# Chained weight loads, a scan behind the logits' transposes, and another order for the sixth unit, in a fused attention and mixture-of-experts kernel

## The chip, the core and the metric

The kernel runs on one core of one Trainium2 chip. The metric is the device time of one launch in microseconds (us), the median of several runs. The core has five engines with a queue of instructions each: PE (TensorE, matmuls), DVE (VectorE), ACT (ScalarE), POOL (GpSimd) and SP (SyncE, which here only issues DMAs). Each takes its own instructions in order and waits on semaphores for the others.

## The reference

Three stages run one after the other, all in float32:

```python
for t in range(S):                       # attention: 4 batches, 8 heads, 768 steps, head size 48
    cur = np.einsum('bhd,bhe->bhde', u[None] * kt, vt)
    y[:, :, t] = np.einsum('bhd,bhde->bhe', rt, state + cur)
    state = wt[:, :, :, None] * state + np.einsum('bhd,bhe->bhde', kt, vt)
# first MLP: 3072 tokens, 384 -> 2048 -> 384
h = x @ w_in
g = h * np.clip(h + 3.0, 0.0, 6.0) / 6.0
x = g @ w_out
# soft mixture: 8 experts with 4 slots each, 384 -> 1024 -> 384
logits = x @ phi
d = softmax(logits, over the tokens);  slot_input = d.T @ x
slot_out[e] = np.maximum(slot_input[e] @ w1[e], 0.0) @ w2[e]
out = softmax(logits, over the slots) @ slot_out
```

## The kernel before

**Units and steps.** The attention is cut into 24 units of 128 time steps of one batch: unit n is chunk n // 4 of batch n % 4. Units 0 to 3 are done ahead of the main loop. The main loop has 96 steps s. Step s does one 128-row tile of the first MLP's hidden layer for a group of four units (512 tokens): g, i = divmod(s, 16), so there are six groups of 16 tiles. Each step has nine matmuls of 512 columns on PE (`mlp`), a relu on ACT (`relu_step`), a product on DVE (`gate`) and a 32x32 block transpose of the product on DVE (`turn_gated`). Between them run four phases of one attention unit per four steps: unit 5 begins in step 1, unit 6 in step 5, and so on to unit 23.

**One unit.** DVE scans the decays from behind (`scan_suffix`) and from the front (`scan_prefix`, behind a small reciprocal, `restart_prefix`). POOL multiplies keys and receptances with them (`decay_keys`, `decay_receptance`), PE makes the scores (`score`), DVE masks them (`mask_scores`), ACT rounds them to 16 bits (`high_scores`), POOL takes the rest (`low_scores`), and PE applies them (`attend`). DVE splits the values (`low_v`) and sums the diagonal (`sum_diag`), POOL applies that (`diag_values`), DVE ends the unit (`finish_y`), and PE transposes the result for the MLP (`turn_x`). Two halves of w_in's rounding rest are made by DVE's `low_w`, the others by POOL's.

**A border.** When a group ends, its logits are folded on PE (`fold_logits`), DVE takes their maximum (`group_maximum`), ACT makes the weights, DVE transposes these (`turn_weight`) and the logits (`turn_logits`), and PE gathers the group into the slots (`gather_slots`, 64 small matmuls). DVE then adds the result up (`add_slots`), which the next group's second `score` waits for. The borders that still carry a unit are those in steps 18, 34, 50 and 66; the fifth, in step 82, carries none.

**What sets the order.** Everything is written out by hand: each engine's block has a loop over s with conditions on the phase, and an engine does its instructions in just that order. SP has one queue for all loads. Behind the last unit's rows it waits for the last `turn_x` and issues w_out and three of the second mixture's W1 tiles at once:

```python
            sp.wait_ge(x_turned, UNITS)
            sp.dma_start(att[:, 0:2 * UNIT], w_out).then_inc(w_out_in, 16)
            for e in range(2, 5):
                sp.dma_start(w1_place[e], w1[e]).then_inc(w1_in[e // 4], 16)
            sp.wait_ge(dg_ready, 16 * (C - 1))
```

w_out is read by PE behind the last group, W1 behind that. The memory that they go into is that of the attention, which is free from then on.

Of the kernel before, what the change touches and what calls it, by code (L numbers as in the profile page):

```python
# [27 lines left out]
C = S // P  # L28
# [20 lines left out]
def build_program(nc, wT, rkT, nat_in_dram, u, u_blocks, w_in, w_outT, w_out, phi, w1, w2, out):  # L49
    with ExitStack() as ctx:  # L50
# [293 lines left out]
        def is_unit(n):  # L344
            return 0 <= n < UNITS
# [10 lines left out]
        def _(sp):  # L356
# [50 lines left out]
                load_rows(n)  # L407
                load_nat(n)
            sp.wait_ge(x_turned, UNITS)
            sp.dma_start(att[:, 0:2 * UNIT], w_out).then_inc(w_out_in, 16)  # L410
            for e in range(2, 5):
                sp.dma_start(w1_place[e], w1[e]).then_inc(w1_in[e // 4], 16)
            sp.wait_ge(dg_ready, 16 * (C - 1))
            for a in range(2):
                sp.dma_start(early[a], w2[EARLY][:, a * UNIT // 2:(a + 1) * UNIT // 2]).then_inc(w2_early_in, 16)
# [42 lines left out]
        def _(pe):  # L458
# [332 lines left out]
                for a in range(4):  # L791
                    fold_earlier(a, half)
            pe.wait_ge(logits_done, C)
            pe.wait_ge(w_out_in, 16)
            for half in range(2):
                for a in range(4):
                    fold_last(a, half)
# [99 lines left out]
        def _(dve):  # L897
# [81 lines left out]
            def low_v(n):  # L979
                dve.wait_ge(v_hi_done, n - B + 1)  # L980
                nc.vector.scalar_tensor_tensor(v_lo[n % 2], nat_of(n, 2), V_SCALE, v_hi[n % 2],  # L981
                                               ALU.mult, ALU.subtract).then_inc(v_lo_done, 1)
# [10 lines left out]
            def gate(s):  # L993
                dve.wait_ge(relu_done, s + 1)
                if s >= GATED:
                    dve.wait_ge(l_ready, 4 * ((s - GATED) // 4 + 1))
                nc.vector.scalar_tensor_tensor(gated_tile(s), relu_tile(s), 6.0 * GATE, hid[s % 2][:],  # L997
                                               ALU.min, ALU.mult).then_inc(gated_done, 1)
# [135 lines left out]
            scan_suffix(B + 1)  # L1134
            restart_prefix(B + 1)
            mask_first(B)
            low_v(B)

            for s in range(END):
                n, phase = unit_of(s)  # L1140
                g, i = divmod(s, FT)
                if s <= 1:
                    gate(s)
                    turn_gated(s)
                if phase == 0:
                    if is_unit(n - 1):
                        finish_y(n - 1)
                    if n - 1 < LAST_INC:
                        add_state(n - 1)
                if phase == 1:  # L1150
                    if 1 <= g < C and i == 2:
                        group_maximum(g - 1)
                    if is_unit(n):
                        mask_scores(n)
                    if is_unit(n + 1):
                        scan_suffix(n + 1)
                        restart_prefix(n + 1)
                    if is_unit(n - 1) and n % B == 0 and n > B:
                        low_x(n - 1)
                    if 1 <= g < C and i == 2:  # L1160
                        turn_weight(g - 1)
                        turn_logits(g - 1)
                    if g == C and i == 2:
                        last_maximum()
                if phase == 2:
                    if g == C and i == 3:
                        turn_weight(C - 1)
                    if g >= 1 and i == 3:
                        sum_weight(g - 1)
                    if is_unit(n - 1) and n % B:  # L1170
                        low_x(n - 1)
                    if is_unit(n):
                        sum_diag(n)
                        low_v(n)
                if s == 0:
                    low_w(1)
                    sum_diag(B)
                if phase == 3:
                    if is_unit(n + 1):
                        scan_prefix(n + 1)  # L1180
                    if s == STEPS + 4:
                        dve.wait_ge(run_sum_done, C)
                        nc.vector.tensor_scalar(run_sum, run_sum, 1e-9, None, ALU.add).then_inc(sum_inv_step, 1)
                        dve.wait_ge(sum_inv_step, 1)
                        nc.vector.reciprocal(run_sum, run_sum).then_inc(sum_inv_step, 1)
                        dve.wait_ge(sum_inv_step, 2)
                        nc.vector.tensor_scalar(fold_inv[:], fold32, run_sum, None, ALU.mult).then_inc(fold_inv_done, 1)
                        dve.wait_ge(fold_inv_done, 1)
                        nc.vector.tensor_scalar(fold_alpha, fold_inv[:], alpha, None, ALU.mult).then_inc(fold_inv_done, 1)
                    if 1 <= g < C and i == 4:  # L1190
                        add_slots(g - 1)
                if s == 4:
                    dve.wait_ge(w_phi_ready, 4)
                    nc.vector.transpose(w_phi[:], l_ps[:]).then_inc(w_phi_done, 1)
                if s == STEPS - 12:
                    cols, tiles = c_parts[0]
                    dve.wait_ge(logits_done, C - 1)
                    nc.vector.tensor_reduce(cmax[:, tiles], by_slot(soft[:, cols]), AX_X, ALU.max).then_inc(c_max_done, 1)
                if s == STEPS - 8:
                    c_inverse(0)  # L1200
                if s == STEPS + 3:
                    copy_cT(1)
                    copy_cT(0)
                if 1 < s < STEPS - 1:
                    gate(s)
                if 1 < s < STEPS - 2:
                    turn_gated(s)
                if s == STEPS - 1:
                    last_gate(0)
                    turn_gated(STEPS - 2)  # L1210
                    last_gate(1)
                    turn_gated(STEPS - 1)
# [270 lines left out]
        def _(pool):  # L1483
# [33 lines left out]
            def low_scores(n):  # L1517
                pool.wait_ge(scores_hi_done, n - B + 1)
                nc.gpsimd.tensor_tensor(scores_lo, scores, scores_hi, ALU.subtract).then_inc(scores_lo_done, 1)  # L1519
# [56 lines left out]
            decay_keys(B + 1)  # L1576
            diag_products(B)
            low_scores(B)
            diag_values(B)

            for s in range(END):
                n, phase = unit_of(s)
                if phase == 0 and is_unit(n):
                    diag_products(n)
                if phase == 1:
                    if is_unit(n):
                        low_scores(n)
                if phase == 2:
                    if n + 1 < UNITS:
                        decay_keys(n + 1)  # L1590
                if phase == 3:
                    if n + 1 < UNITS:
                        decay_receptance(n + 1)
                    if is_unit(n) and n > B:
                        diag_values(n)
                    if n + 1 < UNITS:
                        decay_state(n + 1)
                c = split_behind(s)
                if c is not None:
                    low_w(c)  # L1600
# [73 lines left out]
```

## Time and profile before

| | us |
|---|---|
| median of 3 runs | 425.11 (424.63 to 426.47) |
| the profiled execution | 428.58 |
| its span, first to last instruction | 426.9 |
| PE busy in it | 404.4 |
| DVE busy | 338.4 |
| POOL busy | 188.1 |
| ACT busy | 162.3 |

Busy time of PE counts overlapping matmuls once, and the ends of matmuls are modelled. A profile has each instruction with its start and duration; the time in brackets behind one is what its engine idled just before it, and what is named there ended the idling. "issue" stands where the profile shows nothing that the engine waited for. The profiled execution is 3.47 us over the median of the runs without a profile.

### The profile page before, as it was taken

Reading aid. Unit: us, or ns where it says so; the run is one execution under the profiler, and the core shown is the slowest. Engines: PE = TensorE matmul, PEld = TensorE weight load, DVE = VectorE, ACT = ScalarE, POOL = GpSimd, SP = SyncE. Lnnn points to the kernel's source line nnn. Section 1 sums busy time; section 2 is a strip of 40 time slices with the busy share of each in tenths; the row PEclk is TensorE's granted clock in tenths of the full one; section 3 lists DMA queues with packets and bytes.
Section 4 is the critical chain, followed back from the end, with each engine's and each line's share of the span. In section 5 each row is a group of like instructions: output and inputs, shape, how many; then the busy total and the mean of one; then the engine's idle time right before and its main releaser. Section 6 shows DMA issues by size and latency. Waiting matters only on the chain.

```text
span 426.9 us, 9784 instructions
## 1 busy us (share of the span) xinstructions
PE 404.4 (95%) x3914; PEld 220.9 (52%) x3914; DVE 338.4 (79%) x559; ACT 162.3 (38%) x297; POOL 188.1 (44%) x178
## 2 busy tenths in 40 slices
PE   8998899999999999999999999989999699999981
PEld 4884455555555555556555555445554244543430
DVE  7897799998998989988989988898875847661242
ACT  3586256534234344234441433333333134321242
POOL 4545988874556563465555374725520012010000
PEclk9999999999999999999999999999999989999996
DMA  8999321468033313313440233121009925679929
GB/s 226 321 403 303 124 78 45 122 257 273 11 120 122 97 41 109 122 24 98 122 122 21 103 122 114 51 80 57 2 22 403 382 82 190 211 256 414 401 96 357
DMA packets 16397, 69.35 MB, mean 162 GB/s; under 512 B 2144, under 2 KB 2912, under 8 KB 14688
## 3 DMA queue, kind: packets, MB, share of 16 engines
q1 hardware_dynamic: 16352, 68.73, 46.6%
q8 instruction: 31, 0.51, 0.5%
q14 instruction: 14, 0.11, 0.1%
HBM read 64.00 MB, written 4.72 MB: 161 GB/s over the span
## 4 chain that ended last, share of the span: by engine, by line
issue 34%; PE 31%; POOL 20%; DMA 5%; DVE 5%; ACT 1%; SPq 1%; POOLq 0%; DVEq 0%
POOL att L1528 5%; PE hid L568 4%; PE hid L569 4%; PE hid L570 4%; POOL att L1492 4%; POOL att L1490 3%; DMA att<-rkT_dram 3%; POOL att L1513 3%; POOL att L1546 3%; PE hid L834 2%; PE l_ps L675 2%; POOL w_split L1504 2%; PE y_ps L534 1%; PE hid L815 1%; PE sc_ps L815 1%
## 5 line engine op out<-in xcount | busy, mean ns | idle before, releaser
L1339 ACT ACTIVATE relu<-hid,three 128x512 f32<-128x512 f32 x95 | 65.2, 686 | 142.5 <-PE hid L570 142.2
L568 PE MATMUL hid<-x_split,w_split 128*128 128x512 f16 x285 | 109.0, 382 | 3.2 <-issue 2.8
L569 PE MATMUL hid<-x_split,w_split 128*128 128x512 f16 x285 | 108.6, 381 | 0.0
L570 PE MATMUL hid<-x_split,w_split 128*128 128x512 f16 x285 | 108.5, 381 | 0.0
L997 DVE SCALAR_TENSOR_TENSOR gated<-relu,hid 128x512 f32<-128x512 f32 x95 | 64.5, 679 | 27.9 <-ACT relu L1339 27.2
L1018 DVE STREAM_TRANSPOSE ring<-gated 128x512 f32<-128x512 f32 x96 | 68.3, 711 | 3.3
L1519 POOL TENSOR_TENSOR att<-att 128x1024 f16<-128x1024 f32 x20 | 40.6, 2030 | 48.3 <-ACT att L1274 48.3
L568 PEld LDWEIGHTS hid<-x_split,w_split 128*128 128x128 f16 x285 | 27.8, 98 | 40.1 <-issue 8.5
L1537 POOL TENSOR_TENSOR att<-att 112x512 f32<-112x512 f32 x19 | 22.5, 1183 | 57.0 <-DVE att L916 57.0
L570 PEld LDWEIGHTS hid<-x_split,w_split 128*128 128x128 f16 x285 | 28.0, 98 | 34.2 <-issue 0.8
L569 PEld LDWEIGHTS hid<-x_split,w_split 128*128 128x128 f16 x285 | 28.0, 98 | 25.3 <-issue 0.9
L534 PE MATMUL y_ps<-att 112*128 112x96 f32 x160 | 33.7, 295 | 1.9 <-DVE att L981 1.4
L1528 POOL TENSOR_TENSOR att<-att 112x512 f32<-112x512 f32 x21 | 26.8, 1277 | 10.3 <-DVE att L904 10.3
L470 PEld LDWEIGHTS sc_ps<-att 48*128 48x128 f32 x384 | 23.3, 187 | 11.9 <-issue 11.8
L904 DVE TENSOR_TENSOR_SCAN att<-att 112x517 f32<-112x517 f32 x22 | 28.2, 1280 | 1.5 <-DMA att<-wT_dram 1.3
L470 PE MATMUL sc_ps<-att 48*128 48x128 f32 x384 | 27.9, 284 | 1.3 <-issue 1.3
L675 PE MATMUL l_ps<-ring,soft 32*32 32x512 f32 x192 | 25.4, 594 | 3.0 <-DVE logits L1037 2.2
L534 PEld LDWEIGHTS y_ps<-att 112*128 112x128 f32 x160 | 24.9, 189 | 6.5 <-issue 4.8
L1297 ACT ACTIVATE x_split<-y_ps 128x384 f16<-128x384 f32 x24 | 11.8, 491 | 42.1 <-PE y_ps L551 42.1
L916 DVE TENSOR_TENSOR_SCAN att<-att 112x517 f32<-112x517 f32 x22 | 26.5, 1205 | 0.0
L675 PE MATMUL sc_ps<-ring,soft 32*32 32x512 f32 x384 | 26.1, 598 | 0.0
L1274 ACT ACTIVATE att<-att 128x1024 f16<-128x1024 f32 x20 | 21.1, 1057 | 12.0 <-DVE att L936 11.0
(269 smaller groups left out, 760.2 us busy)
## 6 DMA issues: line engine op xcount, KB each, us to landing
att<-nat_dram SPq DMA_DIRECT2D x20, 576.0 KB, 4.2
att<-rkT_dram SPq DMA_DIRECT2D x22, 448.0 KB, 5.7
att<-wT_dram SPq DMA_DIRECT2D x22, 226.2 KB, 4.8
att<-w_dram SPq DMA_DIRECT2D x3, 1536.0 KB, 16.8
out_dram<-w_split SPq DMA_DIRECT2D x12, 384.0 KB, 3.9
att<-w_dram SPq DMA_DIRECT2D x5, 768.0 KB, 10.2
stage<-w_in_dram SPq DMA_DIRECT2D x2, 1536.0 KB, 15.5
ring<-w_outT_dram SPq DMA_DIRECT2D x1, 3072.0 KB, 17.1
```

What stands on the lines that cost most here:

```text
L470: last = pe.matmul(sc_bank[j][:, cols], k_dec[n % 2][rows, cols], r_dec[n % 2][rows, cols], start=True, stop=True)
L534: pe.matmul(both, r_dec[n % 2][0:PD, p * P:(p + 1) * P], state[b][0:PD, p, :], start=True, stop=False, skip_group_check=True)
L568: pe.matmul(hid[s % 2][:], high, x_high, start=(q == 0), stop=False)
L569: pe.matmul(hid[s % 2][:], high, x_low, start=False, stop=False)
L570: last = pe.matmul(hid[s % 2][:], low, x_high, start=False, stop=(q == KT - 1))
L675: ins = pe.matmul(dg_bank[a][SLOTS * c:SLOTS * (c + 1), :], weight_T[SLOTS * a:SLOTS * (a + 1), b * SLOTS:(b + 1) * SLOTS], ring_group(g, ...
L904: nc.vector.tensor_tensor_scan(suffix[0:PD, ::-1], w_rows_of(n)[0:PD, ::-1], mark[0:PD, ::-1], 1.0, ALU.mult, ALU.add).then_inc(suffix_don ...
L997: nc.vector.scalar_tensor_tensor(gated_tile(s), relu_tile(s), 6.0 * GATE, hid[s % 2][:], ALU.min, ALU.mult).then_inc(gated_done, 1)
L1018: nc.vector.transpose(ring_tile(s), gated_tile(s)).then_inc(gated_turned, 1)
L1339: nc.scalar.activation(relu_tile(s), hid[s % 2][:], ACT.Relu, bias=three[:], scale=GATE / H_SCALE)\
L1519: nc.gpsimd.tensor_tensor(scores_lo, scores, scores_hi, ALU.subtract).then_inc(scores_lo_done, 1)
L1528: nc.gpsimd.tensor_tensor(dst, keys, decay, ALU.mult).then_inc(k_dec_done, 1)
```

## The change

It has four parts.

- **Loads.** w_out is loaded in two halves, and each of the two halves and each of three W1 tiles is issued only when the one before has landed. The wait of `apply_w_out` on PE counts both halves.
- **Borders.** In steps 18, 34, 50 and 66 DVE transposes the weights and logits ahead of the next unit's `scan_suffix` and `restart_prefix`, not behind them.
- **Fifth border.** In step 82 DVE takes the group's maximum ahead of the transpose of step 81's gated tile.
- **Unit 5.** Its `scan_prefix` goes ahead of the main loop on DVE, `low_v(4)` behind the first `gate`, `sum_diag(4)` ahead of `low_w(1)`; on POOL its `decay_receptance` goes ahead of `diag_values(4)`.

```diff
             sp.wait_ge(x_turned, UNITS)
-            sp.dma_start(att[:, 0:2 * UNIT], w_out).then_inc(w_out_in, 16)
+            for half in range(2):
+                cols = slice(half * UNIT, (half + 1) * UNIT)
+                sp.dma_start(att[:, cols], w_out[:, cols]).then_inc(w_out_in, 16)
+                sp.wait_ge(w_out_in, 16 * (half + 1))
             for e in range(2, 5):
                 sp.dma_start(w1_place[e], w1[e]).then_inc(w1_in[e // 4], 16)
+                sp.wait_ge(w1_in[e // 4], 16 * (e % 4 + 1))
             sp.wait_ge(dg_ready, 16 * (C - 1))
...
-            pe.wait_ge(w_out_in, 16)
+            pe.wait_ge(w_out_in, 32)
...
             mask_first(B)
-            low_v(B)
+            scan_prefix(B + 1)
...
                     gate(s)
+                    if s == 0:
+                        low_v(B)
                     turn_gated(s)
...
                     if is_unit(n):
                         mask_scores(n)
+                    if 1 <= g < C and i == 2:
+                        if g == C - 1:
+                            turn_gated(s - 1)
+                        turn_weight(g - 1)
+                        turn_logits(g - 1)
                     if is_unit(n + 1):
                         scan_suffix(n + 1)
                         restart_prefix(n + 1)
                     if is_unit(n - 1) and n % B == 0 and n > B:
                         low_x(n - 1)
-                    if 1 <= g < C and i == 2:
-                        turn_weight(g - 1)
-                        turn_logits(g - 1)
...
                 if s == 0:
+                    sum_diag(B)
                     low_w(1)
-                    sum_diag(B)
                 if phase == 3:
-                    if is_unit(n + 1):
+                    if is_unit(n + 1) and n > B:
                         scan_prefix(n + 1)
...
-                if 1 < s < STEPS - 2:
+                if 1 < s < STEPS - 2 and s != STEPS - FT + 1:
                     turn_gated(s)
...
             low_scores(B)
+            decay_receptance(B + 1)
             diag_values(B)
...
                 if phase == 3:
-                    if n + 1 < UNITS:
+                    if n + 1 < UNITS and n > B:
                         decay_receptance(n + 1)
```

DVE's queue where the main loop begins, before. The rows are the mask of unit 4 (L946), `low_v` (L981), `gate` and `turn_gated` of step 0, `low_w(1)` (L987), `sum_diag` (L977), and unit 5's prefix scan (L916, printed as SCALAR_TENSOR_TENSOR):

```order
L946 TENSOR_TENSOR att<-sc_ps,mask 128x2x256
L981 SCALAR_TENSOR_TENSOR att<-att 128x384 [waits v_hi_done]
L997 SCALAR_TENSOR_TENSOR gated<-relu,hid 128x512 [waits relu_done]
L1018 STREAM_TRANSPOSE ring<-gated 128x512 [waits gated_done]
L987 SCALAR_TENSOR_TENSOR w_split<-stage,w_split 128x2x384 [waits w_hi_done]
L977 TENSOR_REDUCE diag<-att 128x8 [waits diag_v_done,rku_done]
L916 SCALAR_TENSOR_TENSOR att<-att 112x517 [waits r_dec_done,restart_done]
```

And the same place on DVE after the change, where the lines are 4 higher (the scan is L920, `low_v` L985, `low_w` L991):

```order
L950 TENSOR_TENSOR att<-sc_ps,mask 128x2x256
L920 SCALAR_TENSOR_TENSOR att<-att 112x517 [waits r_dec_done,restart_done]
L1001 SCALAR_TENSOR_TENSOR gated<-relu,hid 128x512 [waits relu_done]
L985 SCALAR_TENSOR_TENSOR att<-att 128x384 [waits v_hi_done]
L1022 STREAM_TRANSPOSE ring<-gated 128x512 [waits gated_done]
L981 TENSOR_REDUCE diag<-att 128x8 [waits diag_v_done,rku_done]
L991 SCALAR_TENSOR_TENSOR w_split<-stage,w_split 128x2x384 [waits w_hi_done]
```

The scan moved up by five places, ahead of the first `gate`, and `low_v` to behind that.

POOL's queue at the same place after the change: the two products of `diag_products(4)` (L1498, L1500), `low_scores(4)` (L1527), `decay_receptance(5)` (L1545) and `diag_values(4)` (L1521). Before, the last two stood the other way round:

```order
L1498 TENSOR_TENSOR att<-att 128x384 [waits u_in,nat_in0]
L1500 TENSOR_TENSOR att<-att 128x384 [waits rk_done]
L1527 TENSOR_TENSOR att<-att 128x1024 [waits scores_hi_done]
L1545 TENSOR_TENSOR att<-att 112x512 [waits scores_ready,y_ready,rk_rows_in1,prefix_done]
L1521 TENSOR_TENSOR att<-att,diag 128x384 [waits y_done,diag_done]
```

The receptances of unit 5 no longer stand behind the diagonal of unit 4.

DVE's queue at the border in step 66, before: the mask of unit 21 (L936), unit 22's suffix scan (L904) and reciprocal (L909), the weights' transpose (L1059), the logits' four (L1037), and the next `gate` (L997):

```order
L936 TENSOR_TENSOR att<-sc_ps,mask 128x1024 [waits scores_lo_done,scores_ready]
L904 SCALAR_TENSOR_TENSOR att<-att 112x517 [waits decayed,k_dec_done,w_rows_in2]
L909 RECIPROCAL att<-att 112x4 [waits suffix_done]
L1059 STREAM_TRANSPOSE soft<-soft 128x512 [waits weight_done,dg_ready]
L1037 STREAM_TRANSPOSE logits<-l_ps 32x128 [waits weight_done]
L1037 STREAM_TRANSPOSE logits<-l_ps 32x128 x3
L997 SCALAR_TENSOR_TENSOR gated<-relu,hid 128x512 [waits l_ready,relu_done]
```

After the change, at the same border:

```order
L940 TENSOR_TENSOR att<-sc_ps,mask 128x1024 [waits scores_lo_done,scores_ready]
L1063 STREAM_TRANSPOSE soft<-soft 128x512 [waits weight_done,dg_ready]
L1041 STREAM_TRANSPOSE logits<-l_ps 32x128 [waits weight_done]
L1041 STREAM_TRANSPOSE logits<-l_ps 32x128 x3
L908 SCALAR_TENSOR_TENSOR att<-att 112x517 [waits decayed,k_dec_done,w_rows_in2]
L913 RECIPROCAL att<-att 112x4 [waits suffix_done]
L1001 SCALAR_TENSOR_TENSOR gated<-relu,hid 128x512 [waits l_ready,relu_done]
```

The scan and its reciprocal now stand directly ahead of the `gate`, and the transposes directly behind the mask.

## Rows read from the trace of the kernel before

**Rows 1.** The page: PE's busy time, and the instruction loads by queue.
```profile
PE 404.4 (95%) x3914; PEld 220.9 (52%) x3914; DVE 338.4 (79%) x559; ACT 162.3 (38%) x297; POOL 188.1 (44%) x178
...
q8 instruction: 31, 0.51, 0.5%
```

**Rows 2.** Timeline of PE where it idled: start, us, line, [idle before].
```profile
42.36 0.43 PE L534 MATMUL y_ps<-att 112*128 112x96 f32 x2 [0.50 <-POOL att L1519]
46.49 1.16 PE L470 MATMUL sc_ps<-att 48*128 48x128 f32 x16 [1.25 <-issue]
...
282.74 0.63 PE L675 MATMUL l_ps<-ring,soft 32*32 32x512 f32 x4 [1.12 <-DVE logits L1037]
...
333.36 0.63 PE L675 MATMUL l_ps<-ring,soft 32*32 32x512 f32 x4 [1.13 <-DVE logits L1037]
...
340.62 0.61 PE L568 MATMUL hid<-x_split,w_split 128*128 128x512 f16 x1 [2.81 <-issue]
...
347.18 0.39 PE L568 MATMUL hid<-x_split,w_split 128*128 128x512 f16 x1
```

**Rows 3.** Stretches: length, busy us of PE, PEld, DVE, ACT, POOL, PEclk, DMA share, GB/s.
```profile
307.80:337.90 30.10, 28.88 (x270) 13.26 (x268) 20.07 (x35) 10.00 (x16) 3.52 (x3) 1.00 0.61 253
...
340.60:344.10 3.50, 3.48 (x9) 1.28 (x10) 1.49 (x3) 0.00 (x0) 1.93 (x2) 0.54 0.89 359
```

**Rows 4.** DMA queues from 308 to 337.7 us: packets, MB, share of the engines.
```profile
q1 hardware_dynamic: 528, 7.47, 60.6%
q14 instruction: 3, 0.02, 0.2%
```

**Rows 5.** Timeline of POOL and DVE in unit 6: one held by the other.
```profile
63.05 1.65 POOL L1504 TENSOR_TENSOR w_split<-stage,w_split 128x768 f16<-128x768 f32 x1
64.03 1.76 DVE L904 TENSOR_TENSOR_SCAN att<-att 112x517 f32<-112x517 f32 x1
65.27 2.31 POOL L1519 TENSOR_TENSOR att<-att 128x1024 f16<-128x1024 f32 x1 [0.57 <-ACT att L1274]
```

**Rows 6.** Timeline of DVE and POOL where the main loop begins.
```profile
37.53 0.77 DVE L981 SCALAR_TENSOR_TENSOR att<-att 128x384 f16<-128x384 f32 x1
37.85 1.32 POOL L1490 TENSOR_TENSOR att<-att 128x384 f32<-128x384 f32 x1
40.80 2.22 DVE L987 SCALAR_TENSOR_TENSOR w_split<-stage,w_split 128x768 f16<-128x768 f32 x1
45.22 1.18 POOL L1537 TENSOR_TENSOR att<-att 112x512 f32<-112x512 f32 x1
```

**Rows 7.** Timeline of the borders: step 50's and step 66's, and what idles between.
```profile
218.14 0.69 DVE L997 SCALAR_TENSOR_TENSOR gated<-relu,hid 128x512 f32<-128x512 f32 x1 [0.89 <-ACT relu L1339]
...
233.06 0.86 DVE L1083 SCALAR_TENSOR_TENSOR acc<-acc,stats,k_ps 128x384 f32<-128x384 f32 x2
234.84 1.16 PE L470 MATMUL sc_ps<-att 48*128 48x128 f32 x16
...
279.38 1.23 DVE L904 TENSOR_TENSOR_SCAN att<-att 112x517 f32<-112x517 f32 x1
280.62 2.00 POOL L1519 TENSOR_TENSOR att<-att 128x1024 f16<-128x1024 f32 x1 [3.17 <-ACT att L1274]
...
290.61 0.74 DVE L1083 SCALAR_TENSOR_TENSOR acc<-acc,stats,k_ps 128x512 f32<-128x512 f32 x1
292.77 1.16 PE L470 MATMUL sc_ps<-att 48*128 48x128 f32 x16
```

**Rows 8.** Timeline of DVE at the fifth border.
```profile
328.96 0.71 DVE L1018 STREAM_TRANSPOSE ring<-gated 128x512 f32<-128x512 f32 x1
329.60 0.65 DVE L1028 TENSOR_REDUCE stats<-l_ps 128x1 f32<-128x512 f32 x1
```

**Rows 9.** DVE behind the last full gather, and the landing of one lone 1,536 KB tile.
```profile
341.28 0.81 DVE L1198 TENSOR_REDUCE stats<-logits 128x20 f32<-128x640 f32 x1
...
DMA to landing us min/median/max: 6.2/6.2/6.2
```

## The prediction

> **What bounds the kernel now.** First the busy times: PE has work in 404.4 of 426.9 us, DVE is the next [rows 1]. So what counts is where PE idles, and which other engine has least room behind it. PE's timeline shows the idle places inside the main loop [rows 2]: 0.50 us at 42.36 (the first `attend`, for POOL's L1519), 1.25 at 46.49 (`score(5)`), 1.12 at 282.74 and 1.13 at 333.36 (two gathers, for DVE's transposed logits), and 2.81 at 340.62, ahead of a plain `mlp`, where the profile names nothing. Between 47 and 282 us PE hardly idles: there a change on another engine gains nothing, and costs only once that engine becomes later than PE's slack.
>
> The stretch view tells what 340.62 is. In the 3.5 us behind the idling PEclk is 0.54, so PE ran at about the lower of its two levels (1.2 GHz) after idling 2.8 us; the stretches around it are at 1.00, the 2.4 GHz level [rows 3]. And PE's instructions are fetched by DMA: 31 packets on q8 for 3914 matmuls [rows 1], one for 126. From 307.8 to 337.9 us PE did 270 matmuls [rows 3] without a single q8 packet [rows 4], while SP's queue moved 7.47 MB. It ran out of instructions. The issue that filled the queues is that of w_out and three W1 tiles.
>
> **The change, part by part**
>
> *Loads.* Five transfers of 1,536 KB instead of one of 3,072 and three of 1,536, each issued behind the landing of the last. At most one is outstanding, so a fetch waits for one at most, and PE has room for that: 270 matmuls went by on what one packet and its store gave, some 140 more than the usual 126. Removed: the 2.81 us, and the clock's loss. I take both off by position: the gather ends at 340.62 - 2.81 = 337.81, and the third `mlp` behind it starts at 347.18, 9.37 later [rows 2]. Undisturbed, PE needs 18 matmuls of 512 columns at 2.4 GHz, 3.84, and the logits' two groups of 0.5 each: 4.9. But that `mlp` also needs a `gate` that stands behind DVE's sum and maximum. DVE is through with those at 342.09 [rows 9], 4.28 behind the gather, plus 0.7 for the `gate` and 0.1 for the semaphore: 5.05. Gain 9.37 - 5.05 = **4.3**. What it costs: one tile alone takes 6.2 us to land [rows 9], so five take, with SP's 0.3 between them, 5 x 6.5 = 33 us from 318 (the w_out issue) on, and SP comes free at about 350 instead of 338, some 5 us earlier by the other gains. Behind it stand w2's early parts and W1's fifth tile (issued at 351 before). All are read behind 385 us, so 28 us cover this; cost 0.
>
> *Fifth border.* The maximum (L1028) starts at 329.60 right behind a transpose that starts at 328.96 [rows 8]. With the transpose behind it, the chain maximum, ACT's weights, transposes, gather is 0.64 earlier, and the transpose fits where DVE waited for ACT. PE idles 1.13 there, so all of it counts: **0.65**.
>
> *Four borders.* A plain count would say: the transposes end 1.4 us earlier (scan 1.23, reciprocal 0.18), and PE's 1.12 us in step 66 goes. But something is late instead. When the scan is asked for at 64.03 while POOL's L1504 runs until 64.70, it ends at 65.79, 1.09 behind POOL's end; and L1519, asked for at 65.27, ends at 67.58 [rows 5]. Scans and POOL's products of two SBUF operands don't run side by side; the later one waits for the other's end. Before, the border's scan ran from 279.38 to 280.61, and L1519 began at 280.62 [rows 7]. Behind 1.9 us of transposes the scan is asked for at 281.25, in the middle of L1519, and ends at 282.62 + 1.10 = 283.7. The reciprocal and the next `gate` start 1.24 us later than before, and so does all of DVE behind them.
>
> The Trainium skill (SBUF — State Buffer, Who interferes with whom) says that a DVE instruction with two SBUF inputs contends with a GpSimd instruction that reads SBUF, and that the pair of ports is held for the whole instruction. The rows agree, and by this rule the sum for this part is the one below; without it the part would give 1.1.
>
> Is 1.24 us hidden? The tightest reader is `score`, which waits for DVE's sum. In step 66's group the sum ends at 290.61 + 0.74 = 291.35 and `score` starts at 292.77: slack 1.42; in step 50's the sum ends at 233.92, `score` at 234.84: slack 0.92 [rows 7]. So step 66 gains 1.12 and gives back 1.24 + 1.12 - 1.42 = 0.94; step 50 gives back 0.32 (more if PE gets ahead there too); steps 18 and 34, with the same form, are taken as even. DVE catches up before the next border, where it waited 0.89 us for a relu [rows 7]. Sum 1.12 - 0.94 - 0.32 = **-0.1, taken -0.2**. Bounds: +1.1 (all hidden) and 4 x -1.24 = -5.0 (nothing).
>
> *Unit 5.* `score(5)` waits for POOL's L1537 (45.22 + 1.18 = 46.40) [rows 6], last in the row scan, `diag_values`, `decay_receptance`. Moved up, it is ready by 45.1 (below), and PE could start at 45.24, when it came free: 1.25. But the scan now lies on POOL's products. `low_v` ended at 38.30, and L1490 behind it at 39.17 [rows 6]. The scan, asked for at 37.53, waits for POOL's L1528 to 37.89 (the row just ahead of L1490's) and ends at 38.99; L1490 (0.87 behind a release) then ends at 39.86, L1492 at 40.9. `low_v`, behind the `gate` at 40.1, waits for that and ends at 41.4, and L1519 (65.79 to 67.58, 1.79 behind a release, [rows 5]) ends at 43.15 instead of about 42.2. `attend(4)`, which PE already idled 0.50 for, starts 0.94 later, and PE reaches `score(5)` at 45.24 + 0.94 = 46.2. `low_w` (2.22 long, being held) is released at 43.15 and done by 44.0, L1537 by 45.1: no longer last. Gain 46.49 - 46.2 = **0.3**. Bounds: 1.25, and about -0.9 (`attend` late, and `score` as late again).
>
> **Sum.** 4.3 + 0.65 - 0.2 + 0.3 = 5.05 of the profiled 428.58: 423.5. That execution stands 3.47 over the median of the runs, and I take the same difference off: 425.1 - 5.0 = 420.1.
>
> **The rivals**
>
> *B, everything is hidden.* Holding costs nothing on PE: the borders give 1.1 and up to 0.15 in each of three more gathers, unit 5 gives 1.25. 4.3 + 0.65 + 1.6 + 1.25 = 7.8: 417.3. For it: DVE idles for ACT once a group. Against it: the slacks of 0.92 and 1.42.
>
> *C, the stall stays.* For it: from 20 to 35 us the queues were just as full, and PE was not held there; also the profile itself may load the queues, so the plain runs may have less of a stall to lose. Then 0.65 - 0.2 + 0.3 = 0.75: 424.4. Against it: 270 matmuls without a fetch, and the first one just when the tiles had moved. The Trainium skill (DMA: Bandwidth & Descriptors, Queues, rings and completion order) has each DMA engine take turns between the rows it has work for, a packet at a time. By that rule a fetch would never wait for a row's whole backlog and the chain of loads would change nothing; the trace speaks against it.
>
> *D, DVE becomes the bound (not faster).* Place: the borders. Each has DVE 1.24 us late, and if PE has less slack than at the two `score`s that I looked at, each border costs it in full: -5.0, and at the start -0.9. 4.3 + 0.65 - 5.0 - 0.9 = -0.95: 426.1. It decides from the point at which more than 1.0 us a border and the late start reach PE. Over 427.2 it goes only if lateness is also carried from border to border. Against it: the idle time of 0.89 [rows 7].
>
> **How the numbers follow.** A, the sum above: 0.64. B 0.13, C 0.15, D 0.08. A's own range is 418.8 to 422.0. The range 417.2 to 424.0 takes B in and goes towards C. About 0.5% (2.1 us) is what a measurement of this kernel tells from no change, so faster is below 423.0: A, B and a little of C, 0.78; slower is above 427.2, a part of D: 0.03; the rest 0.19.
>
> **What the profile after would show.** Right: no idle place of over 0.5 us in PE behind the fifth gather, PEclk 1.00 from 330 to 360 us, and q8 packets no more than some 20 us apart; the third `mlp` 5.0 to 5.1 us behind the gather's end. The border's scan 2.3 to 2.5 us long and ending 1.1 behind POOL's L1519 (L1527 now), with the next `gate` 1.2 us later against the mask. PE waiting about 0.9 us at `score(22)` or a neighbour. L1519 of unit 4 ending near 43.1, `score(5)` starting near 46.2. Wrong: a scan that runs beside POOL (then B), a stall that stays or moves to a later `mlp` (then C), PE idling near 1 us at every border (then D), or a wait for w_out or W1 behind 375 us.

## The result, and the profile after

| | before | after |
|---|---|---|
| median, us (16 runs each) | 425.22 (424.63 to 427.75) | 427.20 (426.42 to 431.31) |
| profiled execution, its span | 428.58, 426.9 | 427.10, 425.4 |

The ratio after to before is 1.0058 (95% interval 1.0037 to 1.0079): the change makes the kernel 2.0 us slower. The forecast was 420.1 us. The two profiled executions show the opposite sign, since that of before (428.58 us) was longer than each of the 16 runs in the table. So the comparison of traces has to tell what one execution did from what the kernel does.

The page's first part and PE's waits after, the answer to [rows 1, 2]:

```profile
PE 403.6 (95%) x3914; PEld 219.4 (52%) x3914; DVE 344.4 (81%) x559; ACT 161.7 (38%) x297; POOL 187.9 (44%) x178
...
PE sc_ps L474 <- DVE acc L1087: 2.4, 3, 1.2
PE hid L572 <- issue: 2.0, 1, 2.0
PE y_ps L538 <- DVE att L985: 1.8, 4, 0.5
```

The waits' columns are us in total, times, longest. DVE is busy 6 us longer for the same 559 instructions: it is held. And `score` waits for DVE's sum three times, which before had no such row at all; the last row (`attend` waiting for `low_v`) stood at 1.4 us in three times before. The timeline of PE, in the same form as [rows 2]:

```profile
42.42 0.43 PE L538 MATMUL y_ps<-att 112*128 112x96 f32 x2 [0.60 <-POOL att L1527]
45.23 1.16 PE L474 MATMUL sc_ps<-att 48*128 48x128 f32 x16
...
235.01 1.16 PE L474 MATMUL sc_ps<-att 48*128 48x128 f32 x16 [0.80 <-DVE acc L1087]
...
293.78 1.16 PE L474 MATMUL sc_ps<-att 48*128 48x128 f32 x16 [1.25 <-DVE acc L1087]
302.73 0.43 PE L538 MATMUL y_ps<-att 112*128 112x96 f32 x2 [0.41 <-DVE att L985]
...
334.21 0.63 PE L679 MATMUL l_ps<-ring,soft 32*32 32x512 f32 x4 [0.41 <-DVE logits L1041]
340.69 0.39 PE L572 MATMUL hid<-x_split,w_split 128*128 128x512 f16 x1 [2.03 <-issue]
```

The 1.25 us before `score(5)` and the 1.12 at the fourth gather are gone, and the fifth gather's 1.13 are 0.41. In their place stand 0.80 and 1.25 at `score`, 0.41 at `attend(22)`, and the idling without a name ahead of the plain `mlp` has stayed: 2.03 us.

The border in step 66 on DVE and POOL, as in [rows 7], with the last sum of that group and of step 50's:

```profile
279.08 1.22 DVE L940 TENSOR_TENSOR att<-sc_ps,mask 128x1024 f32<-128x1024 f32 x1
281.46 2.00 POOL L1527 TENSOR_TENSOR att<-att 128x1024 f16<-128x1024 f32 x1 [3.15 <-ACT att L1282]
282.11 2.44 DVE L908 TENSOR_TENSOR_SCAN att<-att 112x517 f32<-112x517 f32 x1
284.80 0.69 DVE L1001 SCALAR_TENSOR_TENSOR gated<-relu,hid 128x512 f32<-128x512 f32 x1
...
233.88 0.87 DVE L1087 SCALAR_TENSOR_TENSOR acc<-acc,stats,k_ps 128x384 f32<-128x384 f32 x2
...
292.78 0.74 DVE L1087 SCALAR_TENSOR_TENSOR acc<-acc,stats,k_ps 128x512 f32<-128x512 f32 x1
```

The scan takes 2.44 us and ends 1.09 behind POOL's product, as forecast. The next `gate` starts 5.72 behind the mask. PE's `score` starts 0.26 behind the sum's end in both groups (233.88 + 0.87 = 234.75 and 235.01; 293.52 and 293.78).

Last the stretch ahead of the idling, in the columns of [rows 3], the load issues, and the queues from 309.7 to 338.3 us and from 338.3 to 339.6 us, as in [rows 4]:

```profile
309.70:338.30 28.60, 28.19 (x269) 13.07 (x267) 19.68 (x35) 9.72 (x15) 3.20 (x3) 1.00 0.47 165
338.40:340.60 2.20, 0.26 (x13) 0.00 (x0) 1.61 (x5) 0.00 (x0) 0.00 (x0) 1.00 0.05 19
340.70:344.20 3.50, 3.50 (x17) 1.61 (x18) 2.88 (x6) 0.69 (x1) 1.18 (x1) 1.00 0.77 270
...
320.22 6.59 SPq L412 DMA_DIRECT2D att<-w_out_dram  x2
332.82 7.95 SPq L415 DMA_DIRECT2D att<-w_dram  x2
...
q1 hardware_dynamic: 418, 4.69, 46.3%
q14 instruction: 3, 0.02, 0.3%
...
q1 hardware_dynamic: 14, 0.02, 5.0%
q8 instruction: 1, 0.02, 4.5%
```

The chain of loads works as written, and no engine waits for w_out or W1, so the cost of 0 that the prediction gave it holds. Still PE went 269 matmuls without a q8 packet, and that packet came at 338.4 us, when the first W1 tile (issued at 332.82) had just stopped moving. The clock stayed at 1.00 (2.4 GHz) this time.

### The profile page after: what moved, and what is told of

Same layout as the page of the kernel before. It is cut to its first block, busy times and chain, and to the rows that moved or that the text cites. A ratio compares the mean times of both kernels' runs of the same rounds, so it can differ in the third digit from the quotient of the medians.

```text
span 425.4 us, 9786 instructions
## 1 busy us (share of the span) xinstructions
PE 403.6 (95%) x3914; PEld 219.4 (52%) x3914; DVE 344.4 (81%) x559; ACT 161.7 (38%) x297; POOL 187.9 (44%) x178
## 4 chain that ended last, share of the span: by engine, by line
issue 36%; PE 27%; POOL 21%; DVE 6%; DMA 5%; ACT 2%; POOLq 0%; SPq 0%; DVEq 0%
DMA att<-rkT_dram 4%; POOL att L1536 4%; POOL att L1498 4%; PE hid L572 4%; POOL att L1500 4%; PE hid L574 4%; PE hid L573 4%; POOL att L1521 3%; POOL att L1554 3%; POOL w_split L1512 3%; PE hid L838 2%; PE l_ps L679 2%; PE hid L819 1%; PE sc_ps L819 1%; PE l_ps L619 1%
## 5 line engine op out<-in xcount | busy, mean ns | idle before, releaser
L1527 POOL TENSOR_TENSOR att<-att 128x1024 f16<-128x1024 f32 x20 | 40.9, 2046 | 46.1 <-ACT att L1282 46.1
L1545 POOL TENSOR_TENSOR att<-att 112x512 f32<-112x512 f32 x19 | 23.2, 1220 | 57.4 <-DVE att L920 57.4
L908 DVE TENSOR_TENSOR_SCAN att<-att 112x517 f32<-112x517 f32 x22 | 32.8, 1490 | 1.4 <-DMA att<-wT_dram 1.3
L920 DVE TENSOR_TENSOR_SCAN att<-att 112x517 f32<-112x517 f32 x22 | 28.2, 1284 | 0.0
```

The lines of the kernel that those rows point to most:

```text
L908: nc.vector.tensor_tensor_scan(suffix[0:PD, ::-1], w_rows_of(n)[0:PD, ::-1], mark[0:PD, ::-1], 1.0, ALU.mult, ALU.add).then_inc(suffix_don ...
```

## The experiments

Each was timed against the kernel before on the same chip. The ratio is not the quotient of the two medians beside it (the change's medians give 1.0047, its ratio is 1.0058); differences in the text are those of the medians, and whether one is clear of noise is judged by the interval.

| kernel | median us | before us | ratio (95%) |
|---|---|---|---|
| e1 loads alone | 424.67 | 425.20 | 0.9974 (0.9950 to 0.9997) |
| e2 four borders alone | 427.88 | 425.20 | 1.0056 (1.0037 to 1.0075) |
| e3 fifth border alone | 424.79 | 425.20 | 0.9990 (0.9971 to 1.0009) |
| e4 unit 5 alone | 424.45 | 425.20 | 0.9986 (0.9964 to 1.0008) |
| s1 238 PE instructions more | 424.41 | 425.40 | 0.9989 (0.9963 to 1.0014) |
| s2 102 PE instructions more | 427.42 | 425.40 | 1.0022 (0.9988 to 1.0056) |
| s3 change without borders | 424.24 | 425.40 | 0.9976 (0.9952 to 0.9999) |
| s4 borders, POOL behind the scan | 426.12 | 425.40 | 1.0029 (1.0008 to 1.0051) |
| r1 all loads behind the gather | 423.30 | 425.07 | 0.9954 (0.9938 to 0.9971) |
| r2 W1 behind the gather | 423.52 | 425.07 | 0.9969 (0.9948 to 0.9991) |
| r3 fifth border, unit 5, loads late | 422.19 | 425.07 | 0.9941 (0.9917 to 0.9965) |
| r4 s3 with s1's instructions | 423.03 | 425.07 | 0.9954 (0.9926 to 0.9983) |
| f1 change with loads late | 425.06 | 425.07 | 1.0014 (0.9986 to 1.0042) |
| f2 r3 with step 66's border | 422.86 | 425.07 | 0.9934 (0.9902 to 0.9966) |

### The four parts, one at a time

Each of e1, e2, e3 and e4 is one of the four parts of the diff above, on the kernel before. In e2 the condition of the moved lines is

```diff
+                    if 1 <= g < C - 1 and i == 2:
+                        turn_weight(g - 1)
+                        turn_logits(g - 1)
```

> The kernel before with the chained loads alone. Theory L (the prediction's first step: PE's 2.8 us before 340.62 come from full load queues): about 4.3 us faster than before in the profile, no PE idling of over 0.5 us before an mlp behind the fifth gather. Theory F (the instruction fetch is late for a reason that the loads have no part in): the idling of 2 to 2.8 us stays in the profile, the instruction packets keep their gap of about 29 us, and the median is within 1 us of before. After the change the idling was still 2.03 us, with at most one transfer outstanding, so F is the likelier.

> The kernel before with the transposes ahead of the scan in steps 18, 34, 50 and 66 alone. Theory D (DVE, held by POOL's product in its scan, becomes later than PE's slack): PE idles 0.3 us at a score near 176, 0.8 near 234, 1.2 near 292 and 0.4 more near 271 and 302, and loses the idling of 1.12 at the fourth gather; together 1.5 to 2.5 us slower than before. Theory A (the prediction's): 0.2 us slower. Theory B (hidden): 1.1 us faster.

> The kernel before with step 82's maximum ahead of the transpose of step 81's tile, and the logits' transposes where they were as to the scan (there is none in that step). By the prediction's step 0.65 us faster: PE idles 0.4 to 0.5 us before the fifth gather and not 1.13. Rival: that gain is taken back behind the gather, where PE waits for a late gate or for its instructions (idling before the next mlp 0.6 longer), then no change.

> The kernel before with unit 5's other order alone. The prediction's step: score(5) starts 0.3 us earlier and the kernel is 0.3 us faster. Rival (the profile after suggests it): PE idles only 0.1 us more at attend(4) and the 1.25 us before score(5) go altogether, and PE is 1.15 us ahead from 50 us on; 1.0 to 1.2 us faster. A second rival: the lead is spent before 100 us, where PE waits for POOL's low_scores of unit 6 or 7, and the time is that of before.

The borders alone lose 2.7 us, theory D; the other three gain 0.5, 0.4 and 0.75 us, the first just outside what its interval leaves to chance, the other two inside. So the sign of the change is that of its borders. They cost a little more than the 1.5 to 2.5 us that theory D had put down, from the waits in the trace of after. PE's waits in e2 are those of after at the same places:

```profile
PE sc_ps L470 <- DVE acc L1083: 2.4, 3, 1.2
PE y_ps L534 <- DVE att L981: 1.8, 4, 0.5
```

PE's idling ahead of the `mlp` behind the fifth gather, by the profiled executions of e1, e2, e3 and e4, in this order:

```profile
337.64 0.39 PE L572 MATMUL hid<-x_split,w_split 128*128 128x512 f16 x1 [0.90 <-issue]
```
```profile
341.54 0.39 PE L568 MATMUL hid<-x_split,w_split 128*128 128x512 f16 x1 [1.27 <-issue]
```
```profile
338.40 0.39 PE L568 MATMUL hid<-x_split,w_split 128*128 128x512 f16 x1 [2.03 <-issue]
...
338.20:341.70 3.50, 3.29 (x9) 1.27 (x10) 2.45 (x6) 0.00 (x0) 0.97 (x1) 0.58 0.97 384
```
```profile
337.70 0.39 PE L568 MATMUL hid<-x_split,w_split 128*128 128x512 f16 x1 [1.44 <-issue]
```

Chained (e1) or not (e2 to e4), it is there, so theory F is right that chaining does not remove it; whether the loads have a part in it is the question of the next section. But with the old loads it is 1.3 to 2.0 us here and not 2.81. After 2.03 us PEclk fell in e3 (0.58, near the 1.2 GHz level), and did not fall after the same 2.03 in the changed kernel. Of the eight profiles that have this idling only two show the fall, before and e3.

### What the late instruction packet hangs on

s1 and s2 add PE instructions ahead of all work, where PE has nothing to do:

```diff
                 for _ in range(n):
-                    pe.matmul(hid[0][:, :], warm[:, 0:P], warm[:, P:P + GT], start=True, stop=True,
-                              skip_group_check=True)
+                    for c in range(8):
+                        cols = slice(c * GT // 8, (c + 1) * GT // 8)
+                        pe.matmul(hid[0][:, cols], warm[:, 0:P], warm[:, P:P + GT // 8], start=True, stop=True,
+                                  skip_group_check=True)
```

> The kernel before, with each 512-column warm-up matmul at the start (17 of them, before PE has any real work) cut into eight of 64 columns: 119 matmuls, 238 instructions of PE more, about one 16 KB packet of q8, and no other difference. Theory I (the late instruction fetch belongs to a place in PE's instruction stream, so it moves to earlier work, where 500 instructions last 27 us): no idling before the mlp behind the fifth gather, PEclk 1.00 there, q8's long gap (540 PE instructions) one packet earlier in the work, by about 13 us; 1 to 3 us faster than before. Rival G (the gather's 128 instructions in 4 us are what the fetch can't follow, wherever the packets' borders lie): the idling of 0.9 to 2.8 us stays where it is and the time is that of before. Rival H (the fetch is held at about 327 us by something else on the chip, at that point of the work): the gap in q8 stays at the same work, and with it the idling.

> The same with four matmuls of 128 columns for each of 512: 51 matmuls, 102 instructions of PE more. Theory I: the late packet is asked for some 5 us earlier in the work, so PE has 102 instructions more of room at the gather; they last longer than the idling of 1 to 2.8 us, so that goes too, and the time is that of the kernel with eight. Rivals G and H: as for that kernel, no change.

In both profiles PE does not idle behind the fifth gather. s1's gain, 1.0 us by the medians, is inside its interval; s2 was no faster, since there a later packet was late, in the last gather:

```profile
375.95 0.61 PE L677 MATMUL sc_ps<-ring,soft 32*32 32x512 f32 x1 [1.80 <-issue]
```

So where the packets' borders lie has a part in it (theory I; by the profiles, since neither interval shows a gain), but theory I's "gap one packet earlier in the work" was wrong: the next packet still began at about 336.8 us in s1, near the gather's end. Something at that point of the work held it, as rival H had it. r1 and r2 ask whether it is the loads:

```diff
+            sp.wait_ge(dg_ready, 16 * (C - 1))
             sp.dma_start(att[:, 0:2 * UNIT], w_out).then_inc(w_out_in, 16)
             for e in range(2, 5):
                 sp.dma_start(w1_place[e], w1[e]).then_inc(w1_in[e // 4], 16)
-            sp.wait_ge(dg_ready, 16 * (C - 1))
```

(r1; in r2 the wait stands behind the w_out line.)

> The kernel before, with w_out and the three W1 tiles issued behind the fifth gather (SP's wait for it moved ahead of them), all at once as before; nothing is loaded from about 318 to 338 us. Theory L2 (a load under way holds the instruction packet that is due at about 328 us, chained or not): the packet comes at 327 to 330 us, 220 to 300 PE instructions behind the one before, PE doesn't idle before the mlp behind the gather, and the kernel is 1 to 3 us faster than before. Theory G2 (loads have no part; that packet only comes when PE has passed the gather): its gap stays over 480 PE instructions and 28 us, PE idles 0.9 us or more there, and the time is that of before, within 1 us. Under both, the load that now runs from 338 to 356 us could hold a later packet instead.

> The kernel before with w_out (3 MB) issued at 318 us as before and the three W1 tiles behind the fifth gather. w_out has landed by about 331 us, before the gather begins at 333. Theory L2: the packet comes at 329 to 332 us, in the gap, PE doesn't idle. Theory G2: as for the kernel with all loads late, no change. If the packet is late in proportion to what is queued, it comes at about 331 us and not at 338.

Theory L2 holds: PE's idling is gone in both, and r1's twelve runs lie within 423.10 to 423.77 us, where those of before reach from 424.43 to 429.22. In r1 the stretch ahead of the packet, the gather's start, and the queues from 333.2 to 334.5 us:

```profile
306.80:333.30 26.50, 25.37 (x176) 11.46 (x174) 17.60 (x31) 10.07 (x16) 3.60 (x3) 1.00 0.00 1
...
332.43 0.63 PE L675 MATMUL l_ps<-ring,soft 32*32 32x512 f32 x4 [1.13 <-DVE logits L1037]
...
q8 instruction: 1, 0.02, 4.7%
```

With nothing in the way, the packet comes about 1 us into the gather, 176 matmuls behind the one before: it isn't 10 us late, as I had read the long gap, but due there. The gather uses 64 matmuls and their weight loads in 4 us, so what is left in PE's store lasts a few us there, and a packet that is held for as long comes too late.

How late it was can be read in the traces (s1, s2 and r4, whose packets' borders lie elsewhere, are left out): the start of the q8 packet behind the gather's first matmul, PE's idling behind the gather, and from the packet's start to the `mlp` that ends the idling, all in us.

| profile | packet behind the gather's start | PE idles | PE goes on behind the packet |
|---|---|---|---|
| e1 (chained) | 3.2 | 0.90 | 2.2 |
| e2 | 3.3 | 1.27 | 2.4 |
| s4 | 3.4 | 1.29 | 2.4 |
| e4 | 3.4 | 1.44 | 2.5 |
| s3 (chained) | 3.9 | 1.72 | 2.3 |
| e3 | 3.9 | 2.03 | 2.6 |
| after (chained) | 4.2 | 2.03 | 2.3 |
| before | 4.8 | 2.81 | 2.5 |
| r1, r2, r3, f1, f2 (no load in flight) | 0.8 to 1.1 | none | |

PE went on 2.2 to 2.6 us behind the packet's start in all eight, and the later the packet, the longer the idling. That is what the profile calls "issue" here. And the delay is the same with the chain (3.2 to 4.2) as without it (3.3 to 4.8): one 1,536 KB tile in flight is enough, and a long backlog is hardly worse.

Nor does the packet wait for the whole backlog. In e3 it started at 335.85, when the queues had moved 7.00 of the 7.86 MB (first line, from 310 to 335.8 us), and the load went on at full rate for two more us while PE stood still:

```profile
q1 hardware_dynamic: 490, 7.00, 65.8%
...
335.80:336.80 1.00, 0.57 (x23) 0.00 (x0) 0.10 (x1) 0.00 (x0) 0.00 (x0) 1.00 0.98 410
336.80:337.80 1.00, 0.00 (x0) 0.00 (x0) 1.00 (x3) 0.00 (x0) 0.00 (x0) 1.00 1.00 399
```

In e2, e4 and s4 it is the same, with 0.8 MB left; only in the trace of before was nearly all moved (7.63 MB).

The Trainium skill (Runtime: NRT & Kernel Launch, Instruction fetch mechanics) says that instructions come in blocks of 256 and that crossing a block is mostly hidden. The size agrees (q8's 31 packets have 0.51 MB); hidden it is not, in a gather with a load in flight: 0.9 to 2.8 us. The same skill (DMA: Bandwidth & Descriptors, Queues, rings and completion order) has the DMA engines take turns between queues. The unchained profiles agree with it so far that the packet did not wait for the backlog's end. In the three chained ones (e1, s3, after) it started just when the tile's data had moved. What order the engines keep between the two queues, and why a load costs the packet 2 to 4 us, stays open.

### The gains put together

s3 is the change without its four borders, r3 the same with r1's loads, r4 is s3 with s1's instructions.

> The change without its four borders (loads, fifth border and unit 5 stay). By the runs of the parts alone: 0.5 + 0.4 + 0.75 = 1.7 us faster than before by the medians, 423.5 us, and 3.7 us faster than the change. If the parts share one gain, since each makes the same idling behind the fifth gather shorter, it is 0.8 to 1.2 us faster than before only.

> The fifth border and unit 5's order of the change, no other border, and all loads behind the fifth gather. Theory L2: the 1.7 us of idling that the kernel without the four borders still showed goes too; 422.3 us, 2.5 to 3 us faster than before. Theory G2: 424.0 to 424.5 us, as with the chained loads.

> The fifth border, unit 5's order and the chained loads of the change, no other border, and the 238 more PE instructions at the start. As with the instructions alone, the packet that was late comes before the gather, and PE doesn't idle behind it: 1.7 us less than without them, 0.2 us more at the start, 422.7 us, 2.0 to 2.8 us faster than before. Rival: the late packet moves on to the dense stretch at 370 to 376 us, as it did with 102 instructions more, and the time is 424 us or more.

s3 gained 1.2 us, not 1.7, and its profile idles 1.72 us behind the gather. r3 is the fastest kernel: 422.19 us, 2.9 us below before and 5.0 below the change. PE's timeline there:

```profile
331.44 0.63 PE L675 MATMUL l_ps<-ring,soft 32*32 32x512 f32 x4 [0.41 <-DVE logits L1037]
335.83 0.39 PE L568 MATMUL hid<-x_split,w_split 128*128 128x512 f16 x1
...
340.83 0.39 PE L568 MATMUL hid<-x_split,w_split 128*128 128x512 f16 x1
```

No idling at 335.83, and the third `mlp` 5.0 us behind the first. r4 gets near it (423.0) and its runs scatter more (422.05 to 426.56): moving the packets works, and is fragile, as s2 shows.

### Why the borders cost so much

s4 takes away the hold: POOL's `low_scores` stays behind the scan.

```diff
                     if is_unit(n):
+                        if n > B + 1 and n % B == 1:
+                            pool.wait_ge(suffix_done, n + 2)
                         low_scores(n)
```

> The four borders alone, as measured before (427.9 us), but POOL's low_scores of these four units waits until the scan has ended. Theory A/D (the scan is late because POOL's product holds it): the scan takes 1.2 us and not 2.4, the next gate is 1.2 us earlier, PE's idling at the four second scores (0.3 to 1.25 us) goes or falls to under 0.2, and the kernel is 2 to 3 us faster than with the borders alone, that is 0 to 1 us faster than before. Rival (DVE is late for the transposes' place by itself, or attend is now late for low_scores): PE idles at score or at attend as before, 427 us or more.

426.12 us: 1.8 of the 2.7 us came back, not all, and `score` still idled 0.34 and 0.81 us in steps 50's and 66's groups, where under 0.2 was expected. The scan is short again, but POOL's next product, now later, holds another DVE instruction, an update of one column that took 0.22 us before:

```profile
223.44 1.23 DVE L904 TENSOR_TENSOR_SCAN att<-att 112x517 f32<-112x517 f32 x1
...
226.71 1.19 POOL L1531 TENSOR_TENSOR att<-att 112x512 f32<-112x512 f32 x1
...
226.95 0.96 DVE L1070 SCALAR_TENSOR_TENSOR stats<-stats 128x1 f32<-128x1 f32 x1
```

So about two thirds of the loss are the hold on the scan (by the starts of the relus, too, 1.9 of e2's 3.0 us). The next one held is in the profile; how much of the rest it makes was not tried.

f1 is the change with r1's loads; f2 is r3 with step 66's border alone moved.

> The whole change with one thing different: the loads all at once and behind the fifth gather, as in the two fastest kernels, not chained ahead of it. If the change's loss is made of two independent parts, the four borders (2.7 us, or 3.2 by the lowest runs) and the 2.0 us of idling behind the fifth gather, this takes 422.2 + 2.7 to 3.2 = 424.9 to 425.4 us, 2 us faster than the change and level with the kernel before. If the borders' lateness runs into the stretch behind the gather, more than that, 426 us.

> The fastest kernel so far (422.2 us: fifth border, unit 5's order, loads behind the gather) with step 66's transposes ahead of the scan as well, the only one of the four whose gather PE waits for (1.12 us). By the progress of the relus in the kernel with all four, this border alone costs 0.74 us net: 422.9 us; PE idles 1.25 us at score(22) and 0.4 near 302, not at the gather. By the prediction's step it gains 1.12 and gives back 0.94: 422.0 us. If the gain is kept because PE is no later at the earlier borders: 421.1 us.

Both came out at the first number given: 425.06 and 422.86 us. The two causes add up: f1 less r3 is 2.9 us for the borders, the change less f1 2.1 for the held packet. And the one border that removes a wait of PE's costs 0.7 by itself. By the runs alone that is inside the intervals of f2 and r3, but the starts of the relus in the two traces give 0.72 as well. Its price is paid in two places:

```profile
291.54 1.16 PE L470 MATMUL sc_ps<-att 48*128 48x128 f32 x16 [1.25 <-DVE acc L1083]
300.50 0.43 PE L534 MATMUL y_ps<-att 112*128 112x96 f32 x2 [0.42 <-DVE att L981]
```

## Why the prediction was wrong

Of the 5.05 us of gain that the sum has, the loads make 4.3 and the borders -0.2, and both were wrong: chaining gave 0.5, the borders took 2.7 to 2.9. Those two differences are most of the 7 us between forecast and result.

**Loads, 4.3 us forecast.** That loads in flight held PE's instruction packet was right. The step that failed is "a fetch waits for one at most, and PE has room for that: 270 matmuls". The 270 matmuls were what PE had done when it had run out, not what was left when the packet fell due. It is due inside the gather, where a stock of instructions lasts microseconds. One tile in flight is too much, and the chain put one exactly there. The other half of the step, that without the chain a fetch waits for the whole backlog, was read off one trace in which the two happened to end together; four others have the packet with 0.8 MB still to move. So the chain had no delay to take away: 3.2 to 4.2 us with it, 3.3 to 4.8 without. The size was off too. Against the profiled 428.58 the estimate is good (r3's third `mlp` stands 5.0 us behind the first, where [rows 2] have 6.56 behind 2.81 of idling), but r1, which removes the idling altogether, gains 1.8 us on the median. One execution's 2.81 us with a clock loss behind it was taken for the kernel's. I had the warning in hand: that execution was 3.47 us over the median, and I took the difference off as a constant, when the stall may well be part of it. The 0.5 us that chaining gave is no proof of a shorter wait either, as the idling varies by 1 us between profiles.

**Four borders, -0.2 forecast, -2.7 to -2.9 measured.** This is the mechanism of rival D, to which I gave 0.08, at somewhat over half of its price of 5.0. The hold itself came as worked out: scan 2.44 us (2.3 to 2.5 forecast), next `gate` 1.33 later against the mask (1.24). What failed is "slack 1.42 ... slack 0.92". The slack was taken from the end of the sum to the start of `score`, but `score` starts at the earliest 0.26 behind that end, so it was 1.16 and 0.66. In step 66 that turns 0.94 of waiting into 1.2, and 1.25 was measured. In step 50 the forecast was 0.32 and 0.80 came. Lateness carried over from the border before is not the reason: the `gate` ahead of this border still idled 0.17 us for its relu, so DVE came to it no later than before. The sum ended 1.34 us later against the mask, PE had got 0.20 ahead at the gather (the case of the prediction's "more if PE gets ahead there too"), and 1.34 + 0.20 - 0.66 = 0.88. And "the tightest reader is `score`" was a count of one: `attend` two steps later waits for `low_v` (0.41 in the row at 302.73). By the starts of the relus that costs 0.35, 0.34, 0.35 and 0.48 us at the four borders, and in all four `attend` starts 0.25 or 0.26 us behind `low_v`'s end. Between steps 50 and 66 a plain `mlp` also waits 0.71 us for its `gate` where it waited 0.43 before; what makes that `gate` late was not traced. Steps 18 and 34, "taken as even", have the cost at `attend` as well, and step 34 0.31 at `score`. By the starts of the relus in the trace of after against that of before, the four borders cost 0.33, 0.57, 1.34 and 0.74 us, 3.0 in all.

**Fifth border, 0.65 forecast.** PE's wait went from 1.13 to 0.41, so 0.72 at its place. Alone it gave 0.4, inside the interval. Whether part of it was given back behind the gather while the packet was late, the rival of e3, is not shown: PE idled 2.03, 1.72 and 2.03 us there with this part (e3, s3, after), and 0.90, 1.27, 1.44, 1.29 and 2.81 without (e1, e2, e4, s4, before), in one profile each. With no packet held, this part and unit 5's gave 1.1 us together (r1 to r3).

**Unit 5, 0.3 forecast.** 0.75 alone, inside its interval too. The traces bear a gain out: by the starts of the relus of steps 0 and 19 the seven profiles with this order gain 0.8 to 1.1 us on that of before, the eight others 0 to 0.6. `score(5)` starts at 45.23 and not 46.2, with no wait. The step that failed is "L1490 (0.87 behind a release) then ends at 39.86, L1492 at 40.9", for which `low_v` would wait and so push L1519's end to 43.15. In the rows after, the first product (L1498) was already running when the scan was asked for. So it held the scan (which ended at 39.20, 1.09 behind it) and was not held itself, and `low_v` ran ahead of POOL's long product:

```profile
37.10 1.01 POOL L1498 TENSOR_TENSOR att<-att 128x384 f32<-128x384 f32 x1
38.19 1.81 POOL L1500 TENSOR_TENSOR att<-att 128x384 f32<-128x384 f32 x1
39.96 2.31 POOL L1527 TENSOR_TENSOR att<-att 128x1024 f16<-128x1024 f32 x1
...
37.20 2.00 DVE L920 TENSOR_TENSOR_SCAN att<-att 112x517 f32<-112x517 f32 x1
...
39.73 0.69 DVE L985 SCALAR_TENSOR_TENSOR att<-att 128x384 f16<-128x384 f32 x1
```

L1527 ended at 42.27 (39.96 + 2.31), so `attend(4)` idled 0.60, 0.1 more than before.

**The whole.** s3's -1.2 and the borders' +2.9 make 425.2 - 1.2 + 2.9 = 426.9, against 427.2 measured. Of C, "the stall stays", I had the time 424.4, and of D 426.1; what happened is both at once, which none of the four cases held. The rival from the Trainium skill's page on DMA, that a fetch never waits for a whole backlog and the chain of loads changes nothing, was nearly right in its result, and e2, e3, e4 and s4 bear out its first half. It does not say why the packet was late all the same; that a load in flight makes it late, the five kernels without one show.

## What to carry to other kernels

A stall that the profile can't name, ahead of dense small instructions, may be a late instruction packet: look at what is in flight when it falls due, and keep big loads out of that stretch altogether rather than spacing them. Measure a slack to the reader's earliest possible start, semaphore included, and list all readers of a late engine before a loss is called hidden. And size a gain by more than one profiled execution when that one lies far from the median.

## What the runs showed of the hardware

- An instruction packet of 16 KB that is due in a stretch of small matmuls stops PE for 0.9 to 2.8 us when a load is in flight, be it one tile of 1.5 MB or the rest of four loads issued at once, and not at all without one (r1, r2, r3, f1, f2). PE goes on 2.2 to 2.6 us behind the packet's start (eight profiles).
- The same 2.03 us of idling was followed by PEclk 0.58 in one profile (e3) and 1.00 in another (after).
- A DVE instruction on one column with both operands in SBUF waits for POOL's running product just as a scan does: 0.96 us for 0.22 (s4).
- A reader on PE started 0.26 us behind the end of the DVE instruction that released it, six times out of six (two `score`s and four `attend`s, 0.25 to 0.26).
